# The low part of the last 64 weight rows, from full-height matmuls to pairs of 64-row matmuls

## The reference

```python
x = einsum('hk,bskhg->bshg', softmax(weight), unfold(x, 7))   # 4 x 4096 tokens, 192 channels, 8 heads
gate = 1.0 / (1.0 + np.exp(-(x @ w_gate)))                    # 192 -> 1536
val = x @ w_val
x = gate * val @ w_out                                        # 1536 -> 192
h = x @ w_in                                                  # 192 -> 2048
r = np.maximum(h, 0.0)
out = (r * r) @ w_out                                         # 2048 -> 192
```

## Time and profile before

| what | value |
|---|---|
| median of 3 runs | 2546.75 us |
| span of the profiled execution, first to last instruction | 2544.7 us |
| TensorE matmul busy | 2511.6 us, 99% of the span, 12420 records |
| TensorE weight load busy | 2154.6 us, 85% |
| VectorE busy | 1830.9 us, 72% |
| ScalarE busy | 1168.7 us, 46% |
| mean granted TensorE clock | 1.000 |
| period of the steady loop body | 78.3 us |

### The profile page before, as it was taken

How to read it: one execution, slowest core, us unless ns; L and a number is a source line. 1 busy time by engine, 2 the same in 40 slices (tenths; PEclk the granted TensorE clock), 3 DMA queues, 4 the chain that set the end, 5 groups by cost and what they waited for, 6 DMA issues and landing times.

```text
span 2544.7 us, 36369 instructions
## 1 busy us (share of the span) xinstructions
PE 2511.6 (99%) x12420; PEld 2154.6 (85%) x12420; DVE 1830.9 (72%) x3618; ACT 1168.7 (46%) x2106; POOL 1.6 (0%) x9
## 2 busy tenths in 40 slices
PE   6999999999999999999999999999999999999999
PEld 4788888888888888888888888888888888888888
DVE  8877677776777776777767777677777677776745
ACT  3544444344444444444444434444444444444444
POOL 0000000000000000000000000000000000000000
PEclk9999999999999999999999999999999999999999
DMA  3100000000000000000000000000000000000000
GB/s 112 40 13 12 0 12 12 12 12 6 6 12 12 12 10 3 12 12 12 12 0 12 12 12 12 6 6 12 12 12 10 2 12 12 12 12 0 7 7 13
DMA packets 39653, 33.44 MB, mean 13 GB/s; under 512 B 1488, under 2 KB 37840, under 8 KB 39632
## 3 DMA queue, kind: packets, MB, share of 16 engines
q1 hardware_dynamic: 39616, 33.17, 4.3%
q10 hardware_dynamic: 16, 0.00, 0.0%
HBM read 20.58 MB, written 12.58 MB: 13 GB/s over the span
## 4 chain that ended last, share of the span: by engine, by line
PE 97%; DVE 2%; issue 0%; DMA 0%; ACT 0%; DVEq 0%; SPq 0%
PE acc L342 15%; PE hp L283 12%; PE hp L284 11%; PE hp L287 11%; PE hp L285 11%; PE hp L286 11%; PE acc L343 7%; PE acc L329 4%; PE acc L325 3%; PE acc L328 3%; PE acc L326 3%; PE acc L327 3%; PE acc L346 1%; DVE xT L594 1%; PE acc L345 0%
## 5 line engine op out<-in xcount | busy, mean ns | idle before, releaser
L567 DVE TENSOR_TENSOR lo<-hid_t,hi 128x512 fp32r<-128x512 f32 x896 | 612.4, 684 | 0.3
L556 DVE TENSOR_TENSOR hid_t<-act_t 128x512 f32<-128x512 f32 x512 | 353.8, 691 | 345.6 <-ACT act_t L443 343.5
L440 ACT ACTIVATE act_t<-hp 128x512 f32<-128x512 f32 x384 | 229.7, 598 | 751.9 <-PE hp L287 751.5
L342 PE MATMUL acc<-wo,hi 128*128 128x384 f32 x1920 | 573.5, 356 | 0.0
L443 ACT ACTIVATE act_t<-hp 128x512 f32<-128x512 f32 x512 | 305.8, 597 | 437.9 <-PE hp L287 436.4
L343 PE MATMUL acc<-wo,lo 128*128 128x192 f32 x1920 | 483.4, 252 | 0.0
L551 DVE TENSOR_TENSOR hid_t<-hp,act_t 128x512 f32<-128x512 f32 x384 | 265.2, 691 | 241.2 <-PE hp L287 236.6
L343 PEld LDWEIGHTS acc<-wo,lo 128*128 128x128 f32 x1920 | 366.3, 191 | 18.7
L342 PEld LDWEIGHTS acc<-wo,hi 128*128 128x128 f32 x1920 | 361.9, 188 | 17.9
L429 ACT CAST hi<-hid_t 128x512 fp32r<-128x512 f32 x512 | 314.9, 615 | 44.4 <-DVE hid_t L556 41.0
L594 DVE STREAM_TRANSPOSE xT<-xin 32x128 f32<-32x128 f32 (+1 forms) x1024 | 275.6, 269 | 31.3
(11 more groups left out here) (79 smaller groups left out, 3741.9 us busy)
## 6 DMA issues: line engine op xcount, KB each, us to landing
xin<-in_x_dram SPq DMA_DIRECT2D x32, 384.0 KB, 3.3
out_dram<-stage SPq DMA_DIRECT2D x32, 384.0 KB, 2.6
stage<-in_moe_w_out_dram SPq DMA_DIRECT2D x7, 384.0 KB, 3.3
stage<-in_moe_w_gate_dram SPq DMA_DIRECT2D x2, 384.0 KB, 4.6
stage<-in_moe_w_gate_dram SPq DMA_DIRECT2D x4, 192.0 KB, 4.3
stage<-in_moe_w_val_dram SPq DMA_DIRECT2D x2, 384.0 KB, 5.3
stage<-in_moe_w_val_dram SPq DMA_DIRECT2D x4, 192.0 KB, 5.3
stage<-in_moe_w_in_dram SPq DMA_DIRECT2D x2, 384.0 KB, 5.2
```

The source lines that it names most:

```text
L342: pe.matmul(both, h, wo2[:, t, :], start=s, stop=False)
L556: dve.tensor_tensor(hid_t[:, t % 4, :], act_t[:, t % 2, :], act_t[:, t % 2, :], ALU.mult).then_inc(sq_done, 1)
L567: dve.tensor_tensor(lo[:, t % RING, :], hid_t[:, t % 4, :], hi[:, t % RING, :].bitcast(F32), ALU.subtract).then_inc(done, 1)
```

## The change

The low part of the last 64 weight rows is no longer multiplied in a full-height matmul. `rest_pair` issues two matmuls of 64 contraction rows instead: the first takes its weights from partitions 0 to 63 of one weight tile, the second from partitions 64 to 127 of another, and they write two different PSUM banks. In the gated stage the two are the gate and the value of tile t, in the squared stage tiles t and t+1, at even t. The pair comes first and starts both banks; `into` then has four matmuls for each bank. For the second matmul the high part of the last 64 activation channels is needed on partitions 64 to 127 too: it goes to a new slot 3 of `xs0` and `xs1`. The product of low weight and low activation is no longer computed. The buffers `y0_hi`, `y1_lo` and `head_of` go; their data are kept in `xs0`, in `y1` and in `act_t`.

```diff
+        xs0 = sb("xs0", [P, 4, N], F32R)
+        xs1 = sb("xs1", [P, 4, N], F32R)
...
+            def rest_pair(dst_a, w_a, c_a, dst_b, w_b, c_b, xs):
+                pe.matmul(dst_a, w_a[0:R, 3, c_a], xs[0:R, 1, :], start=True, stop=False)
+                pe.matmul(dst_b, w_b[R:P, 3, c_b], xs[R:P, 3, :], start=True, stop=False)
             def into(dst, w, xs, t, ready):
                 c = columns(t)
-                pe.matmul(dst, w[:, 0, c], xs[:, 0, :], start=True, stop=False)
+                pe.matmul(dst, w[:, 0, c], xs[:, 0, :], start=False, stop=False)
                 pe.matmul(dst, w[:, 1, c], xs[:, 0, :], start=False, stop=False)
                 pe.matmul(dst, w[:, 0, c], xs[:, 2, :], start=False, stop=False)
-                pe.matmul(dst, w[:, 2, c], xs[:, 1, :], start=False, stop=False)
-                pe.matmul(dst, w[:, 3, c], xs[:, 1, :], start=False, stop=True).then_inc(ready, 1)
+                pe.matmul(dst, w[:, 2, c], xs[:, 1, :], start=False, stop=True).then_inc(ready, 1)
...in1
-                weights_in = prev is None and t % (T1 // 2) == 0
-                if weights_in:
-                    pe.wait_ge(w_lo, split_upto[1 if t == 0 else FIRST + 1])
+                if prev is None and t % (T1 // 2) == 0:
+                    pe.wait_ge(w_lo, split_upto[3 if t == 0 else FIRST + 3])
+                rest_pair(hp[:, 2 * (t % 2), :], wg, columns(t), hp[:, 2 * (t % 2) + 1, :], wv, columns(t), xs0)
                 into(hp[:, 2 * (t % 2), :], wg, xs0, t, gate_ready)
-                if weights_in:
-                    pe.wait_ge(w_lo, split_upto[3 if t == 0 else FIRST + 3])
                 into(hp[:, 2 * (t % 2) + 1, :], wv, xs0, t, val_ready)
...in2
-                if t < 4 and prev[0] == 1:
-                    if t % 2 == 0:
+                if t % 2 == 0:
+                    if t < 4 and prev[0] == 1:
                         pe.wait_ge(prod_done, T1 * prev[1] + T1 - 1 + t // 2)
-                else:
-                    pe.wait_ge(relu_done, T2 * j + t - 3)
+                    else:
+                        pe.wait_ge(relu_done, T2 * j + t - 2)
+                    rest_pair(hp[:, t % 4, :], wi, columns(t), hp[:, t % 4 + 1, :], wi, columns(t + 1), xs1)
...x0_round
-                act.copy(y0_hi[:], y0[:, B:G, :]).then_inc(x0_hi, 1)
                 for half in range(2):
                     act.copy(stacked0[0:R, :, half, :], y0[half * R:(half + 1) * R, B:G, :]).then_inc(x0_hi, 1)
+                for half in range(2):
+                    act.copy(upper0[R:P, :, half, :], y0[half * R:(half + 1) * R, B:G, :]).then_inc(x0_hi, 1)
...x1_round
                 act.copy(xs1[:, 0:2, :], y1[:]).then_inc(x1_hi, 1)
+                act.copy(xs1[R:P, 3, :], y1[R:P, 1, :]).then_inc(x1_hi, 1)
```

More of the change, by code:

```diff
@@ L66, in conv_gated_squared_mlp @@
         stage = sb("stage", [P, STAGES, CHUNK])
-        xs0 = sb("xs0", [P, 3, N], F32R)
-        xs1 = sb("xs1", [P, 3, N], F32R)
+        xs0 = sb("xs0", [P, 4, N], F32R)
+        xs1 = sb("xs1", [P, 4, N], F32R)
         y0 = sb("y0", [P, G, P])
-        y0_hi = sb("y0_hi", [P, B // 2, P], F32R)
         y1 = sb("y1", [P, 2, N])
-        y1_lo = sb("y1_lo", [R, N])
         xin = sb("xin", [P, B, D])
@@ L85, in conv_gated_squared_mlp @@
         stat = sb("stat", [H, 4])
-        head_of = sb("head_of", [H, 2, P])
+        head_of = act_t[0:H, 0, 0:2 * P].rearrange("h (a c) -> h a c", a=2)
         o_sb = stage[:, 0, 0:B * D].rearrange("p (b d) -> p b d", b=B)
@@ L105, in conv_gated_squared_mlp @@
         stacked0 = xs0[:, 1, :].rearrange("p (g h s) -> p g h s", g=B // 2, h=2)
+        upper0 = xs0[:, 3, :].rearrange("p (g h s) -> p g h s", g=B // 2, h=2)
         acc = ctx.enter_context(nc.psum_tensor("acc", [P, 4, 512], F32))
@@ L259, in _ @@
         def _(pool):
-            nc.gpsimd.memset(head_of[:], 1.0).then_inc(heads, 1)
+            nc.gpsimd.memset(head_of, 1.0).then_inc(heads, 1)
             step = 1
@@ L463, in y1_copy @@
                     act.wait_ge(x1_lo, 2 * j)
-                act.copy(y1_lo[:], acc[R:P, 1, :]).then_inc(y1_copied, 1)
+                act.copy(y1[0:R, 1, :], acc[R:P, 1, :]).then_inc(y1_copied, 1)
                 act.copy(y1[:, 0, :], acc[:, 0, :]).then_inc(y1_copied, 1)
@@ L570, in x0_rest @@
             def x0_rest(j):
-                dve.wait_ge(x0_hi, 4 * (j + 1))
+                dve.wait_ge(x0_hi, 5 * (j + 1))
                 m, h = (xs0[:, a, :].rearrange("p (b s) -> p b s", b=B) for a in (2, 0))
@@ L576, in x0_rest @@
                     q = slice(half * R, (half + 1) * R)
-                    dve.tensor_tensor(stacked0[R:P, :, half, :], y0[q, B:G, :], y0_hi[q, :, :].bitcast(F32),
+                    h = (stacked0, upper0)[half][q, :, half, :]
+                    dve.tensor_tensor(stacked0[R:P, :, half, :], y0[q, B:G, :], h.bitcast(F32),
                                       ALU.subtract).then_inc(x0_lo, 1)
             def x1_rest(j):
-                dve.wait_ge(x1_hi, j + 1)
+                dve.wait_ge(x1_hi, 2 * (j + 1))
                 dve.tensor_tensor(xs1[:, 2, :], y1[:, 0, :], xs1[:, 0, :].bitcast(F32), ALU.subtract) \
@@ L618, in y1_add @@
                 dve.wait_ge(y1_copied, 2 * j + 2)
-                for p0 in (0, R):
-                    dve.tensor_tensor(y1[p0:p0 + R, 1, :], acc[0:R, 1, :], y1_lo[:], ALU.add) \
+                for p0 in (R, 0):
+                    dve.tensor_tensor(y1[p0:p0 + R, 1, :], acc[0:R, 1, :], y1[0:R, 1, :], ALU.add) \
                        .then_inc(y1_added, 1)
```

## The result

The changed kernel takes 2664.92 us (median of 4 runs, 2664.87 to 2665.53) where the kernel before took 2546.71 in the same comparison: ratio 1.0465, interval 1.0452 to 1.0478. It is 118 us slower. The prediction was 2455 us with a range of 2400 to 2640, so it was wrong in its sign, and the time lies outside its range. The rival in which each change of height drains the array had been priced at 2660 us.

What follows compares the result with a forecast made beforehand. TensorE was taken as the bound, at 0.23 us a matmul. 640 pairs saving 0.15 us each give 96 us: 2544.7 - 96 + 4 for start-up = 2452.7, plus 2.05 to the median, 2455 us; range 2400 to 2640.

Steps and rivals of the forecast that it cites:

- The rival in which each change of height drains the array: At L281 and the first L287, matmuls wait for earlier ones: 2583 or 2660 us; chance 0.28 for drain over break-even.
- no charge for the changes: At each change between 128 and 64 rows around a pair, the forecast added nothing to the pair's 0.31 us.
- the bound from above: Most a pair could cost: halves one after the other, 0.46, plus 0.26 at each of two changes, 0.98 us.
- break-even of 0.46: What two full-height matmuls of a pair cost before, 2 x 0.23 us; a dearer pair makes the kernel slower.
- The rival on the slower side: Each change of height around a pair drains TensorE, 0.10 or 0.16 us a change: 2583 or 2660 us; chance 0.28.
- the stagger of 0.08: Within a pair, the second half begins 0.08 us after the first, so a pair costs 0.31 us.
- The rival of one step for a pair: Both weight loads are done before the first half starts; a pair costs 0.23 us, total 2406 us; chance 0.20.
- What the gain meets: Four places where something else might be late; only `y1_add` in the squared stage was close, 0.16 us to spare.
- Start-up: First matmul waits for value weights until 26.9 us; with the first two gated stages, 4 us are lost.
- the second stretch of the earlier trace: Taken to show the first two gated stages, with TensorE busy 63.22 of 68.07 us and VectorE 60.15.
- a short drain: Rival: each change of height costs 0.02 to 0.07 us, total 2480 to 2541 us; chance 0.12.
- The count: Pairs in the whole kernel: 384 in gated tiles and 256 in squared tiles, together 640.

Runs made afterwards that it cites:

- k2: The changed kernel with both 64-row matmuls of each pair put into the same half, rows 0 to 63: 2801.39 us, ratio 1.1001 to the kernel before.
- k4: The changed kernel with each pair issued twice in a row, four 64-row matmuls: 2805.58 us, ratio 1.1017 to the kernel before.
- k1: The changed kernel with the two matmuls of each pair made full-height again, same order, copies and waits: 2548.39 us, ratio 1.0007 to the kernel before.
- k11: The changed kernel without pairs, each bank starting with its own single 64-row matmul, 1280 visits: 3047.03 us, ratio 1.1966 to the kernel before.
- k7: The kernel before with single pairs in the squared stage alone, gated stage unchanged: 2588.92 us, ratio 1.0167.
- k3: The changed kernel with the second matmul of each pair left out: 2651.51 us, ratio 1.0412 to the kernel before.
- k8: The changed kernel regrouped so that two pairs are issued together everywhere, in both stages: 2663.83 us, ratio 1.0461 to the kernel before.

## Why the prediction was wrong

- **The step that failed** is "no charge for the changes, since the nearest rows (matmuls of other sizes and other banks following each other) show none". Those rows have no change of height in them, so they were no evidence on it. The charge is 0.415 us a visit, 266 us over 640 visits, where I had 0; it is within the bound from above (2 x 0.26 us), which I had worked out and then not weighed.
- **The step that was mis-sized in the other direction**: the second half starts 0.00 us after the first, not 0.08. That is worth 51 us. Together: 0.23 + 0.41 = 0.64 us a pair where I had 0.31, and a break-even of 0.46.
- **The rival on the slower side was right that each change has a price, and nearly right in its sum.** It had 0.31 + 2 x 0.16 = 0.63 us a pair. Its parts were off and made up for each other: the stagger of 0.08 isn't there, and a change costs 0.21 us, being both of the things that I had put up as alternatives: a wait ahead of the change, of 0.10 us and not 0.16, and 0.10 for the restart behind it. k2 and k4 show them apart. That the sum came within 5 us of the measurement is luck. The restart looks like the one of the earlier trace rows: the same 0.50 us record, the same 0.33 us to the next, and there too the weight load starts with its matmul (33.67 and 33.68), so its price was readable in the trace of before. The Trainium skill (TensorEngine Tiling (Array Packing), Key Properties) says that changing the mode drains TensorE; the trace agrees in so far as both changes of every visit have their wait. That the array empties in it is not shown: the pair at 1301.93 starts before the modelled end (1302.00) of the record ahead of it. I gave this rival 0.28 and should have given it most of the chance, since the only statement on such a change that I had, and the only restart in the rows, both pointed to it.
- The rival of one step for a pair was right in its own step, the halves start together (0.00 to 0.01 us apart), and wrong in its time for the missing charge. That agrees with the 4 ns of the Trainium skill (TensorE: Matmul & The Clock Gate, Part 3: Packing small matmuls) as far as 0.01 us can tell. Its other half, loads taken ahead of matmuls, holds inside a form (k4, where the loads of both halves are 0.24 us ahead) and not over a change: the 640 loads at L287 all started with their matmul.
- **What the gain meets**: there was no gain to meet anything. TensorE doesn't wait for `y1_add`, and the waits for products are 2.8 us instead of 4.7. Whether `y1_add` would be late behind faster pairs stays open.
- **Start-up**: the first matmul starts at 27.25 us (26.9 forecast), and the first product at 31.86 where I had the value ready at 30.8. The 4 us allowed are more than k1 shows, which has the same waits and copies with full-height pairs: 1.9 us. In the changed kernel 640 x 0.187 + 1.9 = 121.6 us stands against 118.2 measured; VectorE paces part of the first two gated stages and may hide the rest there, which no run singles out.
- **Slips that decided nothing**: the second stretch of the earlier trace rows ends at 92.73 us and the second gated stage only at 113.66, so it shows one and a half stages and not two; 30.8 - 29.47 is 1.3 us, not 1.4; and a short drain of 0.07 us a change gives 2544 us, not 2541.
- **The count** of 640 pairs, the step of 0.23 us, and the absence of other causes held: k1 brings the time back to 1.9 us above before.

## What to carry to other kernels

A matmul of 64 rows beside another costs one step for two, but in this kernel the stretch of such matmuls cost about 0.41 us on top, at every place between full-height ones that was tried. Count the changes of form, not the matmuls saved, and put at least two pairs into each stretch; that needs their banks free together, which must be looked up in the trace tile by tile. And when the trace shows nothing on an operation, neighbours that lack its special feature do not bound it.

## What the runs showed of the hardware

- A change between 128-row and 64-row matmuls costs TensorE 0.10 us ahead of it and 0.10 us behind its first matmul, with 192 and with 512 columns ahead, in both directions; two changes together 0.39 us (k11, and the squared stage in k7) to 0.43 us (gated stage), 0.415 us in the mean of the changed kernel.
- The weight load of the first matmul after a change starts with that matmul and not with the one ahead. In the changed kernel this is so at all 640 changes back to full height and at the 639 changes to 64 rows that stand in a running stream.
- Two 64-row matmuls in different halves, into different banks, start within 0.01 us and cost 0.02 us more than one (k3).
- A distance of 2.14 us between starts (k8) was followed, in 23 of 29 cases, by steps of 0.43 us (the lower level, 1.2 GHz); in the case shown for 3.5 us, at a granted clock of 0.56. In six cases the clock stayed at 1.00, as it did behind all 29 distances of 1.33 us.
- Not tried: keeping a whole stage in 64-row form. Both halves of every sum would then have to be added up in one bank, and no run here shows what two halves do in one bank.
